# A retention layer and two MLP layers in one kernel: a reordered prologue, first sums on VectorE, a reordered first quad, and other places for the second layer's first down weights and the last rows

## The reference

```python
# retention: batch 4, heads 8, sequence 768, head dim 64
for t in range(S):
    state = gamma[None, :, None, None] * state + np.einsum('bhd,bhe->bhde', k[:, :, t], v[:, :, t])
    y[:, :, t] = scale * np.einsum('bhd,bhde->bhe', q[:, :, t], state)
x = y.transpose(0, 2, 1, 3).reshape(B * S, H * D)      # 3072 x 512
# layer 1: w_in 512 x 2048, w_out 2048 x 512
h = x @ w_in;  x = (h * np.cos(h)) @ w_out
# layer 2, the same shapes
h = x @ w_in;  g = np.where(h >= 1, h, np.where(h <= -1, 0, (h + 1)**2 / 4));  out = g @ w_out
```

## Time and profile before

| What | Value |
|---|---|
| median of 3 runs | 1090.5 us |
| the profiled execution | 1089.99 us |
| its span in the trace | 1088.2 us |
| PE busy | 1074.1 us, 99% of the span |
| DVE busy | 677.5 us, 62% |
| ACT busy | 517.3 us, 48% |
| POOL busy | 226.1 us, 21% |
| DMA, share of the 16 engines (queue q1) | 38.2% |
| mean granted TensorE clock | 0.998 |

### The profile page before, as it was taken

The page is one execution under the profiler, slowest core; times in us unless marked ns, Lnnn a source line. Parts: engine busy times, 40 slices in busy tenths (PEclk is TensorE's granted clock), DMA queues, the critical chain, the costliest instruction groups (busy, mean ns, idle before and its releaser), DMA issues.

```text
span 1088.2 us, 14491 instructions
## 1 busy us (share of the span) xinstructions
PE 1074.1 (99%) x5574; PEld 886.9 (82%) x5574; DVE 677.5 (62%) x1029; ACT 517.3 (48%) x846; POOL 226.1 (21%) x270
## 2 busy tenths in 40 slices
PE   7999999999999999999999999999999999999998
PEld 5778888887888888788887888888888888888887
DVE  4877674566666455666656766636766636766632
ACT  5687763236665323665664544444332344332332
POOL 4777722300000230000150677400000000000000
PEclk9999999999999999999999999999999999999999
DMA  9445553433332442432253633650422350422111
GB/s 343 155 184 213 211 201 130 146 117 136 136 111 98 160 146 87 156 111 99 81 194 91 269 133 146 223 184 1 173 92 113 136 184 1 162 103 113 68 39 39
DMA packets 44596, 149.12 MB, mean 137 GB/s; under 512 B 4720, under 2 KB 5104, under 8 KB 42480
## 3 DMA queue, kind: packets, MB, share of 16 engines
q1 hardware_dynamic: 44528, 148.20, 38.2%
HBM read 106.24 MB, written 41.94 MB: 136 GB/s over the span
## 4 chain that ended last, share of the span: by engine, by line
PE 91%; DVE 3%; ACT 3%; SPq 1%; issue 1%; DMA 1%; POOL 0%; DVEq 0%; ACTq 0%
PE bank L526 13%; PE bank L528 13%; PE bank L530 13%; PE bank L559 8%; PE bank L560 8%; PE bank L561 8%; PE bank L555 8%; PE bank L556 8%; PE bank L557 8%; PE bank L432 2%; PE bank L459 2%; PE bank L455 1%; PE bank L477 1%; DMA raw<-in_w1u 1%; ACT work L1054 1%
## 5 line engine op out<-in xcount | busy, mean ns | idle before, releaser
L526 PE MATMUL bank<-x_hi,tw 128*128 128x512 f32 x672 | 262.1, 390 | 2.7 <-ACT work L1027 1.3
L530 PE MATMUL bank<-x_hi,tw 128*128 128x512 f32 x672 | 261.6, 389 | 0.0
L528 PE MATMUL bank<-x_lo,tw 128*128 128x512 f32 x672 | 261.6, 389 | 0.0
L555 PE MATMUL bank<-g_hi,wd_hi 128*128 128x512 f32 x384 | 152.4, 397 | 2.1 <-DVE g_lo L793 2.1
L526 PEld LDWEIGHTS bank<-x_hi,tw 128*128 128x128 f32 x672 | 126.1, 188 | 30.4 <-issue 3.2
L556 PE MATMUL bank<-g_lo,wd_hi 128*128 128x512 f32 x384 | 149.7, 390 | 0.0
L557 PE MATMUL bank<-g_hi,wd_lo 128*128 128x512 f32 x384 | 149.7, 390 | 0.0
L560 PE MATMUL bank<-wd_lo,g_hi 128*128 128x512 f32 x384 | 149.5, 389 | 0.0
L559 PE MATMUL bank<-wd_hi,g_hi 128*128 128x512 f32 x384 | 149.5, 389 | 0.0
L561 PE MATMUL bank<-wd_hi,g_lo 128*128 128x512 f32 x384 | 149.5, 389 | 0.0
L530 PEld LDWEIGHTS bank<-x_hi,tw 128*128 128x128 f32 x672 | 126.2, 188 | 26.2
(11 more groups left out here) (96 smaller groups left out, 1393.9 us busy)
## 6 DMA issues: line engine op xcount, KB each, us to landing
tw<-t_scratch SPq DMA_DIRECT2D x64, 896.0 KB, 6.3
t_scratch<-tw SPq DMA_DIRECT2D x16, 1792.0 KB, 7.5
work<-x_scratch SPq DMA_DIRECT2D x24, 256.0 KB, 3.5
raw<-in_w1u SPq DMA_DIRECT2D x16, 256.0 KB, 3.2
wd_raw<-in_w1d SPq DMA_DIRECT2D x8, 512.0 KB, 8.7
q_sb<-in_q_t SPq DMA_DIRECT2D x16, 256.0 KB, 2.7
k_sb<-in_k_t SPq DMA_DIRECT2D x16, 256.0 KB, 3.7
v_sb<-in_v_n SPq DMA_DIRECT2D x16, 256.0 KB, 3.0
```

The lines of the kernel that those rows point to most:

```text
L526: nc.tensor.matmul(to[:, :], w[:, kt, 0, i, :], x_hi[:, i, kt, :], start=opens, stop=False, skip_group_check=True)
L528: nc.tensor.matmul(to[:, :], w[:, kt, 0, i, :], x_lo[:, i, kt, :], start=False, stop=False, skip_group_check=True)
L530: last = nc.tensor.matmul(to[:, :], w[:, kt, 1, i, :], x_hi[:, i, kt, :], start=False, stop=kt == 1, skip_group_check=True)
L555: nc.tensor.matmul(to[i][:, :], wd_hi[:, f, cols], g_hi[:, slot, :], start=opens, stop=False)
```

## The change

Prologue. PE's warm-up reads the first state tile and waits for one memset instead of two. PE does `outputs(u)`, `outer(u)`, `scores(u + 2)`. On DVE `mask(1)` goes ahead of `scale_q(2)`. On ACT `copy_state(0)` goes ahead of `scale_k(1)`. SP issues the first up weights behind `q` and `k` of `u` = 6, two loads later. The sums 0 and 1 of the first up weights go from POOL to DVE, behind `mask(5)`. POOL does `scale_q` 3 to 7 in a row, then `t_low` 0 and 1, `t_sums` 2 and 3, both `first_x3`, their two low parts, `t_low(2)`, `t_low(3)`. On ACT `t_high(0)` and `t_high(1)` go behind units 4 and 5, `t_high(2)` behind the loop, `t_high(3)` and `wd_high(0, 0)` into the first quad.

The last sums. On DVE the two sums of `kt` = 1 go ahead of the low parts of `kt` = 0. On ACT `copy_p1(0, 0)` goes behind the high parts of p5 and p3.

First quads. In all spans `sum_h21` goes ahead of `gate_low`, and `sum_h12` ahead of `gate(1)`; in span 0 `update_state(7)` and `angle(0)` go to the front.

Layer 2's first down weights are split in the first quad of span 3, on ACT behind the copies of rows and on POOL ahead of its other work; `wd_low` steps its semaphore once for each of its two instructions.

The end. The second and fourth last rows go by DVE, the fourth in two column halves, whose second is stored from ACT's queue. The first scores of a span wait for two row copies less.

```diff
@@ sync
-                if u == 5:
-                    load_weights(0)
+                if u == 6:
+                    load_weights(0)      # now behind load_k(u)
...
-            store_rows(SPANS - 1, 2)
+            s, chunk = SPANS - 1, C - 1
+            for i in range(3):
...
+            sp.wait_ge(last_rows_done, 2)
+            sp.dma_start(out_rows[3, chunk][:, HALVES[0]], late[:, ROWS_2[3], HALVES[0]]).then_inc(rows2_out[3], 16)
@@ tensor
-                        pe.wait_ge(rows1_done, 4 * (u // AHEAD))
+                        pe.wait_ge(rows1_done, 4 * (u // AHEAD) - 2)
-                    pe.wait_ge(wdlo_done, QUADS * layer + f % QUADS + 1)
+                    pe.wait_ge(wdlo_done, 2 * (QUADS * layer + f % QUADS) + (1 if f < QUADS else 2))
-            pe.wait_ge(zeroed, 2)
+            pe.wait_ge(zeroed, 1)
             for u in range(AHEAD - 2):
                 outputs(u)
+                outer(u)
                 scores(u + 2)
-                outer(u)
@@ vector
+            def first_t_sums(kt):
+                w = raw[0][:, kt, 1, :, :]
+                dve.wait_ge(raw_in[0][kt], 16)
+                nc.vector.tensor_tensor(w[:, 4, :], w[:, 1, :], w[:, 0, :], ALU.subtract).then_inc(t_summed, 1)
...
                     split_low(s, "p4", kt)
+                    if s == 0:
+                        x_sum(s, "s2", 1)
+                        x_sum(s, "s1", 1)
...
                 if q == 0:
                     gate(s, q, 0)
+                    sum_h21(s, q)
                     gate_low(s, 1, q)
                 angle(s, q, 1)
...
+                else:
+                    sum_h12(s, q)
+                    gate(s, q, 1)
...
+                if u == KT - 1:
+                    first_t_sums(0)
+                    first_t_sums(1)
@@ scalar
                     split_high(s, "p4", kt)
+                    split_high(s, "p6", kt)
+                    split_high(s, "p5", kt)
                     if i == 7 and s == 0:
                         split_high(s, "p3", 0)
                         copy_p1(0, 0)
                         split_high(s, "p3", 1)
...
+            def last_rows():
+                for i in (0, 2):
+                    act.wait_ge(rows_ready, i + 1)
...
+                act.wait_ge(last_rows_done, 3)
+                act.dma_start(out_rows[3, C - 1][:, HALVES[1]], late[:, ROWS_2[3], HALVES[1]]).then_inc(rows2_out[3], 16)
...
+                if q == 0 and s == PAIRS:
+                    wd_high(1, 0)
...
+                if u == 4:
+                    t_high(0)
                 if u == 5:
+                    t_high(1)
                     scale_k(7)
-                if u in (3, 4, 5):
-                    t_high(u - 3)
-            t_high(3)
-            wd_high(0, 0)
+            t_high(2)
@@ gpsimd
-            for u in range(3, 6):
+            for u in range(3, AHEAD):
                 scale_q(u)
-            t_sums(0)
-            t_sums(1)
-            scale_q(6)
-            scale_q(7)
             t_low(0)
             t_low(1)
             t_sums(2)
             t_sums(3)
-            t_low(2)
             first_x3(0)
             first_x3(1)
+            first_x3_low(0)
+            first_x3_low(1)
+            t_low(2)
...
+                    if q == 0 and s == PAIRS:
+                        wd_low(1, 0)
...
-                    wd_low(1, 0)
```

More of the change, by code:

```diff
@@ L72 @@
 LAST_OF = {half: max(n for n, item in enumerate(DOWN) if item[0] == half) for half in (1, 2)}
+HALVES = [slice(0, D // 2), slice(D // 2, D)]
 ROWS_2 = [QUADS - 2, FT - 2, QUADS - 1, FT - 1]
@@ L319, in store_rows @@
                 for i in range(4):
[L320 to L323, removed]
+                    sp.wait_ge((rows1_done, rows2_done)[half - 1], 4 * s + i + 1)
                     tile = work[:, X21 + i, :] if half == 1 else late[:, ROWS_2[i], :]
@@ L388, in _ @@
                         load_wd(1, q)
-            store_rows(SPANS - 1, 2)
+            s, chunk = SPANS - 1, C - 1
+            for i in range(3):
+                if i == 1:
+                    sp.wait_ge(last_rows_done, 1)
+                else:
+                    sp.wait_ge(rows2_done, 4 * s + (1 if i == 0 else 2))
+                sp.dma_start(out_rows[i, chunk], late[:, ROWS_2[i], :]).then_inc(rows2_out[i], 16)
+            sp.wait_ge(last_rows_done, 2)
+            sp.dma_start(out_rows[3, chunk][:, HALVES[0]], late[:, ROWS_2[3], HALVES[0]]).then_inc(rows2_out[3], 16)
             for i in range(4):
                 sp.wait_ge(rows1_out[i], 16 * SPANS)
-                sp.wait_ge(rows2_out[i], 16 * SPANS)
+                sp.wait_ge(rows2_out[i], 16 * (SPANS if i < 3 else SPANS + 1))
         @block.tensor
@@ L568, in warm_up @@
                 for _ in range(count):
-                    nc.tensor.matmul(banks[7][:, :], state[:, 1, 0, :], state[:, 1, :, :].rearrange("p b t -> p (b t)"),
+                    nc.tensor.matmul(banks[7][:, :], state[:, 0, 0, :], state[:, 0, :, :].rearrange("p b t -> p (b t)"),
                                      start=True, stop=True)
-            pe.wait_ge(zeroed, 2)
+            pe.wait_ge(zeroed, 1)
             warm_up(WARM_UP)
@@ L739, in operands @@
                         gate_low(s - 1, *lows.pop(0))
-                    x_sum(s, "s2", kt)
-                    x_sum(s, "s1", kt)
                     if s:
+                        x_sum(s, "s2", kt)
+                        x_sum(s, "s1", kt)
                         x3_sum(s, kt)
@@ L851, in quad @@
                     finish(s, q - 1)
+                if s == 0 and q == 0:
+                    update_state(AHEAD - 1)
+                    angle(s, q, 0)
                 sum_u2(s, q)
@@ L858, in quad @@
                     sum_u3(s, q)
-                angle(s, q, 0)
+                if s or q:
+                    angle(s, q, 0)
                 if q:
@@ L862, in quad @@
                     gate(s, q, 0)
-                if s == 0 and q == 0:
-                    update_state(AHEAD - 1)
                 sum_h22(s, q)
@@ L871, in quad @@
                     gate_low(s, 1, q)
-                gate(s, q, 1)
-                sum_h21(s, q)
-                sum_h12(s, q)
+                    gate(s, q, 1)
+                    sum_h21(s, q)
+                    sum_h12(s, q)
+                else:
+                    sum_h12(s, q)
+                    gate(s, q, 1)
             dve.wait_ge(table_first, 16)
@@ L880, in _ @@
             mask(0)
+            mask(1)
             dve.wait_ge(table_rest, 16)
             scale_q(2)
-            mask(1)
             for u in range(AHEAD):
@@ L921, in _ @@
                                 split_low(s + 1, name, kt)
-            for i in (2, 3):
-                dve.wait_ge(rows_ready, i + 1)
-                nc.vector.tensor_copy(late[:, ROWS_2[i], :], up_banks(SPANS - 1)[i][:, :]).then_inc(last_rows_done, 1)
+            dve.wait_ge(rows_ready, 2)
+            nc.vector.tensor_copy(late[:, ROWS_2[1], :], up_banks(SPANS - 1)[1][:, :]).then_inc(last_rows_done, 1)
+            dve.wait_ge(rows_ready, 4)
+            for part in HALVES:
+                nc.vector.tensor_copy(late[:, ROWS_2[3], part], up_banks(SPANS - 1)[3][:, part]).then_inc(last_rows_done, 1)
         @block.scalar
@@ L1078, in rows_second @@
             def rows_second(s):
[L1079 to L1083, removed]
-                    nc.scalar.activation(late[:, ROWS_2[i], :], up_banks(s)[i][:, :], ACT.Copy).then_inc(rows2_done, 1)
+                act.wait_ge(down_done, ND * (s + 1))
+                for i in range(4):
+                    nc.scalar.activation(late[:, ROWS_2[i], :], up_banks(s)[i][:, :], ACT.Copy).then_inc(rows2_done, 1)
+            def last_rows():
+                for i in (0, 2):
+                    act.wait_ge(rows_ready, i + 1)
+                    nc.scalar.activation(late[:, ROWS_2[i], :], up_banks(SPANS - 1)[i][:, :], ACT.Copy).then_inc(rows2_done, 1)
+                act.wait_ge(last_rows_done, 3)
+                act.dma_start(out_rows[3, C - 1][:, HALVES[1]], late[:, ROWS_2[3], HALVES[1]]).then_inc(rows2_out[3], 16)
             def finish_turns(s, q):
@@ L1109, in quad @@
                 turns(s, q, 0)
+                if s == 0 and q == 0:
+                    t_high(3)
                 curve(s, q, 0)
+                if s == 0 and q == 0:
+                    wd_high(0, 0)
                 if more:
@@ L1124, in _ @@
                 operands(0, u)
+                if u == 0:
+                    copy_state(u)
                 if u < 6:
                     scale_k(u + 1)
-                if u < KT:
+                if 0 < u < KT:
                     copy_state(u)
+                if u == 4:
+                    t_high(0)
                 if u == 5:
+                    t_high(1)
                     scale_k(7)
-                if u in (3, 4, 5):
-                    t_high(u - 3)
-            t_high(3)
-            wd_high(0, 0)
+            t_high(2)
             for s in range(SPANS):
```

(6 more changed lines are left out.)

13 lines of the change are left out of this document (6 added, 7 removed).

## The result

The changed kernel takes 1087.12 us, median of 6 runs (1086.06 to 1087.68), the kernel before 1090.51 us (6 runs). The ratio is 0.9964 with a 95% interval of 0.9953 to 0.9974: 3.9 us faster by the ratio, somewhere from 2.8 to 5.1. The forecast was 1087.0. A second measurement of the same kernel, beside others, gave 1087.38 (0.9965, 0.9951 to 0.9979). The profiled execution took 1087.68 us, the slowest of the six, so its profile shows 0.56 us more than the median has.

What follows compares the result with a forecast made beforehand. PE, busy 1074.1 of 1088.2 us, bounds the kernel, so only its waits can be won. 1.1 + 0.86 + 0.3 + 1.24 = 3.5 us off 1089.99 gives 1086.5; median 0.5 above, 1087.0; 8-in-10 range 1084.4 to 1088.8.

Steps and rivals of the forecast that it cites:

- The stall goes, p1 at 34.4: Prologue: PE's 2.48 us wait for POOL's scaled Q and 1.5 us of slow clock vanish; p1 starts at 34.4, not 38.35.
- p2 is late next, at 41.2: First quad: p2 waits for copy_p1 behind a line over DVE, ACT and POOL, starting at 41.2 instead of 37.2.
- The clock falls again, 1.5 us: First quad: PE idles 4.0 us before p2, so the slow clock is charged 1.5 us again.
- Gain 1.1 before the second quad, 0.3 more in span 0: Second quad starts at 49.8 instead of 50.9, gaining 1.1 us; span 0's wait for a gate goes, 0.3.
- the forecast's own sign that the prologue lost: Profile after: a second quad starting later than 51 would mean that the prologue lost.
- just in time: Second quad: POOL's line delivers the low part of the next weights at about 49.4.
- First quads 0.86: First quads of later spans: two waits of PE for g_lo, 0.43 us each, go; 0.86 us gained.
- Layer 2's weights 1.24: Tail of span 2: PE's wait at 573 for g_lo goes once the weight split moves to span 3; 1.24 us.
- The end 0: Last rows: storing the last row in halves, the second from ACT's queue, gains 0 us.
- The slower rival: End: ACT's store of the last half row lands after 8.3 us instead of 2.1, giving 1093.2; chance 0.06.
- prologue pays nothing: Prologue: late weights, or port meetings and slow clock, eat the 1.1 us; 1088.1 in all; chance 0.2.
- the two later terms: After span 0: the g_lo waits in first quads, 0.86 us, and layer 2's first down weights, 1.24 us.

Runs made afterwards that it cites:

- e6: The changed kernel with 18 more matmuls of 128x512, output unread, between p7 and p2 in PE's idle time: 1085.83 us, ratio 0.9953.
- e8: The changed kernel unchanged, timed and profiled again beside others on the same chip: 1087.38 us.
- e1: The kernel before with only the prologue, the last sums and span 0's first quad as changed: 1090.24 us, ratio 0.9994.
- e2: The kernel before with only the order of sum_h21 and sum_h12 changed in the first quads of spans 1 to 5: 1089.87 us, ratio 0.9992.
- e3: The kernel before with only layer 2's first down weights split in span 3's first quad, and the split semaphore: 1089.49 us, ratio 0.9986.
- e11: The kernel before with two float32 matmuls, output unread, ahead of scores(6) in PE's wait for POOL's scaled Q: 1091.8 us, ratio 1.0006.
- e12: The changed kernel with a reordered first quad and both halves of wd_low(0, 0) on POOL held until DVE's second angle: 1083.57 us, ratio 0.9923.

## Why the prediction was right

The time was met to 0.1 us, but by errors that cancel. The forecast took 3.5 us off the profiled execution; from profile to profile 2.3 were won. The prologue and span 0 came 2.3 short of their 1.4, the later spans won 3.3 where 2.1 were forecast, and the end lost 0.1. The last 1.1 us is luck of the executions: the forecast put the median 0.5 above its sum, and the profiled execution of after lay 0.56 above its median. Its steps, against the profiled execution:

- *The stall goes, p1 at 34.4*: 34.05. Right. The weights landed in time for DVE's first sum at 22.97; the eight sums took 1.95 us and not 2.4 (0.28 each, starting 0.2 apart).
- *p2 is late next, at 41.2, behind the line over t_high(1), POOL's sums and `first_x3`*: 41.69, and 41.26 and 40.80 in the two other profiles with this prologue. Right, with its cause: POOL's last two sums took 0.94 and 0.90 where 0.46 is normal, and both `first_x3` 3.38 where two are 2.6, while DVE made four low parts in 4.07.
- *The clock falls again, 1.5 us*: right in kind (e6), wrong in size. In before it fell while PE did short matmuls of the retention; here it fell on the twelve matmuls of 128x512 of p2 and p6, which lost 5.25 - 2.85 = 2.4.
- *Gain 1.1 before the second quad, 0.3 more in span 0*: **this step failed.** The second quad started at 51.09 and not at 49.8; beyond 51 was the forecast's own sign that the prologue lost. These 1.3 us are PE's own: p2 was 0.5 late, the slow clock 0.9 dearer, and the rest 0.1 shorter. No wait stands between p2 and the first down product, which came 0.17 later than in before. Then the wait of 0.25 at 68.69 stayed, and one of 0.45 at 61.35, 0.7 by the steps, was added. It is the end of DVE's chain: the slow clock delayed p6, so DVE's first sum had to wait for it (1.27 us, until 47.21); then `gate_low` met `wd_low(0, 0)` and took 1.27 us, where in before it took 0.69 behind it. The forecast had charged the clock to PE alone, and had called POOL's line "just in time" without looking at what its last piece does to DVE. In place of 1.4 us the profile has a loss of 0.9, e8's a loss of 0.5, and the part alone (e1) a gain of 0.65 within -0.3 and 1.5.
- *First quads 0.86*: the two waits went. By the profiles they were worth more: 0.67 each by the steps, 1.8 between the landmarks of e2's profile. The runs have about 0.9 (0 to 1.9) and don't tell. The forecast took the view's idle time for the cost.
- *Layer 2's weights 1.24*: 1.5 in e3 (0.5 to 2.5), 1.55 by its profile. The same reason.
- *The end 0*: two stores of 128 KB landed 2.0 after their issues, also the one from ACT. From the last matmul's start to the span's end it was 3.63 us in before and 3.74 now. The slower rival, a late landing from ACT's queue, didn't come.

The rival "prologue pays nothing" describes the prologue better than the forecast did. Its 1088.1 was wrong: it took the two later terms at 2.1 us where the profile has 3.3, and it put the median 0.5 above the profiled execution like the forecast.

## What to carry to other kernels

When a stall in front of a saturated TensorE is removed, follow the line that the next wait hangs on, over all engines, and price the clock in the matmuls that stand behind the new wait: the same fall is free where another wait hides it (e11) and cost 1.5 us where none does (e6). The idle time of a view is less than what a wait costs TensorE; compare start-to-start steps (0.40 in the view, 0.67 by the steps). An operation of VectorE with two SBUF inputs on the chain is worth keeping clear of GpSimd where the chain has no slack behind it, if need be with a wait on GpSimd (e12: the angle took 0.68 instead of 1.77, and the median was 1.0 us lower, in another set).

## What had not been expected of the hardware

- Eighteen matmuls, 4.2 us, whose output nobody reads made the kernel 1.5 us faster (e6_filled).
- The kernel before is faster in some executions than in others by up to 3 us (1090.04 to 1093.1). In the experiments all its executions at a mean clock of 0.997 took 1091.4 or more, those at 1.00 took 1090.1 to 1091.1, and those at 0.998 lie on both sides. Its prologue was profiled in several kernels, with and without the fall at 26 us: in e2_quads, which has the same prologue, no fall came at all (span 1086.6) though PE had idled 2.81 us, longer than the 2.48 of before; in e3_wd one held over 26 to 34 us (span 1089.9).
- A wait of 0.40 us in the records cost 0.67.
